# An mLSTM, dense and routed layer kernel on one core: one block's table scatters, one slot's rows and one slot's second layer put at other places of their queues

## What is computed

```
# 1. gated recurrent attention, 4 x 8 heads, 768 steps, head size 40
C = f * C + i * outer(v_t, k_t);  n = f * n + i * k_t
y_t = sigmoid(o_t) * (C @ q_t) / max(|n . q_t|, 1)
# 2. dense layer on x = y as 3072 tokens x 320
h = x @ w_in                        # 320 -> 2048
g = where(h >= 1, h, where(h <= -1, 0, (h + 1)**2 / 4))
x2 = g @ w_out                      # 2048 -> 320
# 3. routed layer: each token goes to the best of 8 experts
e = argmax(x2 @ w_gate);  p = softmax(x2 @ w_gate)[e]
out = p * (relu(x2 @ w1[e]) @ w2[e])   # 320 -> 1024 -> 320
```

## Time and profile before

| | |
|---|---|
| median of 3 runs | 816.65 us (814.5, 816.65, 816.67) |
| the profiled execution | 823.59 us, its span 821.4 us |
| PE busy in the span | 768.7 us (94%) |
| DVE, ACT, POOL busy | 595.2 (72%), 422.9 (51%), 318.5 us (39%) |
| PE clock, mean of the span | 0.988 of full |

### The profile page before, as it was taken

The page is one execution under the profiler, slowest core; times in us unless marked ns, Lnnn a source line. Parts: engine busy times, 40 slices in busy tenths (PEclk is TensorE's granted clock), DMA queues, the critical chain, the costliest instruction groups (busy, mean ns, idle before and its releaser), DMA issues. The chain is left out here.

```text
span 821.4 us, 17203 instructions
## 1 busy us (share of the span) xinstructions
PE 768.7 (94%) x5765; PEld 746.8 (91%) x5765; DVE 595.2 (72%) x1009; ACT 422.9 (51%) x649; POOL 318.5 (39%) x297
## 2 busy tenths in 40 slices
PE   2789999999999999999999999988979899999994
PEld 1788999999999999999999999988979899999994
DVE  4653768787878787878878788648677857676751
ACT  3022545454545454545454545663466766666761
POOL 3341543545343434454544444541434141313111
PEclk9999999999999999999999999998989999999998
DMA  6962222222222222222323210566647554338400
GB/s 198 308 174 75 75 93 76 90 75 90 74 90 74 90 74 93 81 95 85 94 87 92 83 40 1 174 160 171 236 145 228 205 198 158 121 94 266 148 7 5
DMA packets 41458, 97.05 MB, mean 118 GB/s; under 512 B 6936, under 2 KB 24482, under 8 KB 39755
## 3 DMA queue, kind: packets, MB, share of 16 engines
q1 hardware_dynamic: 37498, 87.46, 34.0%
q0 software_dynamic: 3920, 9.08, 3.6%
HBM read 105.63 MB, written 9.33 MB: 140 GB/s over the span
## 5 line engine op out<-in xcount | busy, mean ns | idle before, releaser
L552 POOL TENSOR_TENSOR g_t<-u_t,r_t 128x512 f32<-128x512 f32 x96 | 135.7, 1414 | 257.0 <-ACT u_t L702 256.9
L697 ACT ACTIVATE r_t<-bank,neg 128x512 f32<-128x512 f32 x96 | 66.0, 688 | 189.9 <-PE bank L1446 189.9
L1458 PE MATMUL bank<-wo_h,g_h 128*128 128x328 f32 x384 | 127.2, 331 | 0.0
L1033 DVE TENSOR_SCALAR u_t<-bank 128x512 f32<-128x512 f32 x96 | 66.1, 688 | 76.2 <-ACT r_t L697 49.2
L1458 PE MATMUL bank<-wo_h,g_l 128*128 128x328 f32 x384 | 120.2, 313 | 0.0
L1458 PE MATMUL bank<-wo_l,g_h 128*128 128x328 f32 x384 | 120.1, 313 | 0.0
L634 POOL DMA_INDIRECT out_x<-ob,idx_tok x31 | 37.4, 1208 | 153.8 <-ACT ob L772 149.5
L702 ACT ACTIVATE u_t<-u_t,half 128x512 f32<-128x512 f32 x96 | 69.5, 724 | 39.6 <-DVE u_t L1033 38.0
L969 DVE TENSOR_TENSOR_SCAN W<-W,cst 128x512 f32<-128x512 f32 x48 | 83.2, 1737 | 5.0 <-DMA W<-decays 5.0
L1579 PE MATMUL bank<-w_h,h_h 128*128 128x320 f32 x248 | 79.4, 320 | 7.4 <-DVE w_l L1097 6.3
L1446 PE MATMUL bank<-xT_h,wi_h 128*128 (+1 forms) x384 | 79.5, 289 | 1.6 <-issue 1.6
(11 more groups left out here) (234 smaller groups left out, 1949.9 us busy)
## 6 DMA issues: line engine op xcount, KB each, us to landing
raw<-in_w SPq DMA_DIRECT2D x10, 1280.0 KB
W<-decays SPq DMA_DIRECT2D x24, 512.0 KB, 5.0
raw2n<-in_w SPq DMA_DIRECT2D x9, 1280.0 KB
raw<-in_w SPq DMA_DIRECT2D x10, 1024.0 KB
raw1n<-in_w SPq DMA_DIRECT2D x9, 1024.0 KB
raw<-in_w SPq DMA_DIRECT2D x20, 256.0 KB
raw1n<-in_w SPq DMA_DIRECT2D x18, 256.0 KB
qG<-in_q SPq DMA_DIRECT2D x24, 180.0 KB
```

Source lines behind the costliest of these rows:

```text
L552: pool.tensor_tensor(g_t[p % 2][:, :], u_t[p % 2][:, :], r_t[p % 2][:, :], ALU.add).then_inc(sm["g_done"], 1)
L697: act.activation(r_t[p % 2][:, :], bank_h[p % 2][:, :], ACT.Relu, bias=neg1[:, 0:1]).then_inc(sm["r_done"], 1)
L1033: dve.tensor_scalar(u_t[p % 2][:, :], bank_h[p % 2][:, :], 1.0, -1.0, ALU.min, ALU.max).then_inc(sm["u_done"], 1)
L1458: mm = pe.matmul(bank_acc[tt][:, 0:DL], l[p % 4][:, c], r[:, f, :], start=f == 0 and a == 0, stop=f == NT1 - 1 and a == 2)
```

## The change

Three orders are changed; no instruction is added, removed or resized.

1. **Scatters of block 10.** `to_table(10)` stood behind `gated(11, 7)`, the last of POOL's eight sums of the last block. It stands behind `gated(11, 6)` now, ahead of that sum. In all other blocks it stays.
2. **Slot 3 and slot 4.** The second layer of slot 2 was divided into tiles 0 to 2, 3 to 5 and 6 to 7 around `turn_y(3)` and `first2(3)`, `turn_y(4)`. It is divided into 0 to 2, 3 to 4 and 5 to 7. On DVE `y_low(4)` goes ahead of `h_low(3, 3)`.
3. **Slot 6.** On ACT and on DVE the split of its rows (`y_high(6)`, `y_low(6)`) goes ahead of the split of its first weights (`w1_high(6, .)`, `w1_low(6, .)`).

```diff
@@ POOL, body
                     if not att and p in (4, 5):
                         gather(p - 4)
-                if prev:
+                    if not att and p == 6:
+                        to_table(t - 1)
+                if prev and att:
                     to_table(t - 1)
@@ ACT
             h_high(5, 3)
+            y_high(6)
             w1_high(6, 0)
             w1_high(6, 1)
             for s in range(5, NS):
...
-                if s + 1 < NS:
+                if 6 < s + 1 < NS:
                     y_high(s + 1)
@@ DVE
             w1_low(4, 0)
+            y_low(4)
             h_low(3, 3)
-            y_low(4)
             w1_low(4, 1)
...
             h_low(5, 3)
+            y_low(6)
             w1_low(6, 0)
             w1_low(6, 1)
             for s in range(5, NS):
-                if s + 1 < NS:
+                if 6 < s + 1 < NS:
                     y_low(s + 1)
@@ PE, tail
                 turn_y(3)
-                second2(2, range(3, 6))
+                second2(2, range(3, 5))
                 first2(3)
                 turn_y(4)
-                second2(2, range(6, NT2))
+                second2(2, range(5, NT2))
                 first2(4)
```

## The result

The changed kernel took 811.49 us (median of 13 runs, 809.33 to 816.3) beside 817.2 us for the kernel before (13 runs, 814.5 to 823.08). The ratio is 0.9929, with a 95% interval of 0.9908 to 0.995: faster by 0.7%, 5.7 us. Forecast were 8.4 us and 808.3 us. The time lies inside 804.5 to 812.5 us, to which the prediction gave some 8 in 10 and more, and 1.0 us above the narrower 806 to 810.5 us that stands with the forecast. On two other chips the ratio was 0.9921 and 0.9919. The recorded execution went from 821.4 us of span to 814.1, by 7.3 us.

What follows compares the result with a forecast made beforehand. PE, busy 94% of the span, bounds the kernel, so its waits and half-clock stretches count. Gains of 5.5 + 2.7 + 0.2 + 0.0 = 8.4 us take 816.65 to 808.3 us (806 to 810.5; wider 804.5 to 812.5).

Steps and rivals of the forecast that it cites:

- Where part 1 acts, and how: Block 10's scatters start at 537.99 and 539.30; `second2(0)` starts without waiting at 552.3, not 557.83: 5.5 us gained.
- The delay of `gated(11, 7)`: On POOL this sum starts at 540.4, not 539.77, and PE loses the 0.6 us; bounds 0 and 1.7 us.
- The landing: Block 10's scatters must land by 549.4; at 7.7 us they land at 547.0, 2.4 us to spare.
- The rival of a late landing: Block 10's scatters still take 12.34 us and land at 551.6; 810.5 us, or 813.2 with the clock lost; chance 0.11.
- the slower one: Landing set by SP's loads, POOL's issues delay PE 1.7 us, more half clock at slot 3; 819.3 us; chance 0.03.
- The clock behind `second2(0)`: Without the wait ahead of `second2(0)` the clock stays at 2.4 GHz there: 2.7 us gained.
- The size of the wait: The profiled 6.1 us wait of `second2(0)` and its half-clock stretch were taken as gains of 5.5 and 2.7 us.
- a clock lost at slot 6: The broken wait around `first2(6)` loses the clock, costing one more stretch of 2.9 us; 811.2 us; chance 0.10.
- The cost of recording: The profiled execution lies some 7 us above the median, taken as recording cost, the same for both kernels.
- Part 2: Slots 3 and 4: `first2(3)` waits 3.7 us without gain or loss; gain at `first2(4)` capped at 0.2 us.
- Part 3: Slot 6: the 2.4 us wait breaks into about 0.4, 1.9 and 0.8 us; gain 0.0, up to 0.6 us.
- the case that before loses its clock at this wait in other runs: Slot 6: some runs of before lost the clock there and the broken wait keeps it; 805.5 us; chance 0.06.

Runs made afterwards that it cites:

- split kernel: Changed kernel with the second scatter of block 10 issued behind `gated(11, 7)`, the first ahead of it; 804.98 us (ratio 0.9895) and 804.58 us (0.9900) on two chips.
- after, again: The changed kernel, unedited, run once more on a second chip; 807.22 us beside 813.38 us for the kernel before, ratio 0.9921.
- Part 2 alone: Kernel before with only the orders of slots 3 and 4 changed; 811.82 us beside 811.7 us, ratio 0.9996.
- part 3 alone: Kernel before with only the order of slot 6 changed; 811.02 us beside 811.7 us, ratio 0.9982.
- after, third: The changed kernel, unedited, run on a third chip; 805.56 us beside 812.41 us for the kernel before, ratio 0.9919.
- part 1 alone: Kernel before with only the scatters of block 10 moved; 807.58 us beside 811.7 us, ratio 0.9933.
- split without parts 2 and 3: Kernel before with one scatter of block 10 ahead of `gated(11, 7)`, one behind, slots 3, 4 and 6 unchanged; 807.15 us, ratio 0.9938.
- the load behind: Kernel before with SP's load of the first weights of slot 1 issued behind the store of block 11; 812.56 us beside 813.38 us, ratio 0.9981.

## Why the prediction was right, and where it was off

**Where part 1 acts, and how: right.** POOL's scatters at 538.23 and 539.54 (forecast 538.0 and 539.3), 0.82 us after `pair_ready` (535.77 + 1.64 = 537.41), as forecast; no idle time at the copy into `pair`; `second2(0)` at 552.32 (forecast 552.3), at the full clock, with 48 products in 7.2 us. The second scatter began inside `g_low(11, 6)`, took 1.08 us and ended 0.85 us behind it (540.62 and 539.77), which is what the prediction had taken over from the long issue.

**The delay of `gated(11, 7)`: 1.15 us, not 0.6.** From the first product of `first(11, 7)` it starts 539.77 - 534.97 = 4.80 us later in before and 540.65 - 534.68 = 5.97 us later in after, and `second2(0)` 17.65 in place of the 16.50 of the split kernel. My step counted the two issues and took `pair_ready` over unchanged. It comes 2.73 us after that first product in after and 2.20 in before, so it is later by 0.5 us, and the cause lies 5 us upstream. POOL and DVE, before:

```profile
531.17 1.30 POOL L552 TENSOR_TENSOR g_t<-u_t,r_t 128x512 f32<-128x512 f32 x1
532.62 0.97 POOL L581 DMA_INDIRECT xg<-x_scratch,idx_tok  x1 [0.15 <-issue]
...
535.85 1.29 POOL L552 TENSOR_TENSOR g_t<-u_t,r_t 128x512 f32<-128x512 f32 x1 [0.62 <-ACT u_t L702]
```

```profile
531.18 1.32 DVE L1072 TENSOR_SCALAR ssum<-ssum 128x2 f32<-128x2 f32 x1
...
532.62 1.79 DVE L1091 TENSOR_TENSOR w_l<-raw,w_h 128x1536 fp32r<-128x1536 f32 x1
```

The same in after:

```profile
530.88 1.33 POOL L552 TENSOR_TENSOR g_t<-u_t,r_t 128x512 f32<-128x512 f32 x1
532.36 2.44 POOL L581 DMA_INDIRECT xg<-x_scratch,idx_tok  x1 [0.15 <-issue]
```

```profile
530.88 0.17 DVE L1075 TENSOR_SCALAR ssum<-ssum 128x2 f32<-128x2 f32 x1
...
532.20 1.76 DVE L1094 TENSOR_TENSOR w_l<-raw,w_h 128x1536 fp32r<-128x1536 f32 x1 [0.96 <-ACT w_h L730]
```

In before DVE's tiny `ssum` step starts 0.01 us behind POOL's sum and is held until that ends (532.50 and 532.47). In after it starts with the sum, takes 0.17 us, and so `w1_low` comes 0.16 us ahead of the gather and not with it, and the gather's issue takes 2.44 us. POOL's next sum is late by that, and the conversion into `dsti` is held until it ends: 1.64 us, to 537.41, where the sum ends at 536.07 + 1.30 = 537.37. In before it is held as well, for 0.96 us to 537.17, where the sum ends at 537.14. So `pair_ready` was never a time of DVE's own. In all thirteen profiles it comes 0.02 to 0.04 us behind the end of `gated(11, 6)`, and what delays that sum delays the scatters. All six profiles with both scatters ahead of the sum have this long gather and the conversion of 1.64 us, all seven of the other kernels have a short gather and 0.95 or 0.96 us, on all chips. Why the two engines meet 0.01 us differently at a place that the change does not touch, the runs do not say. In the recorded execution it did not show in `second2(0)`, and that 552.3 was met to 0.02 us is luck: the dense layer happened to be 0.3 us sooner (534.68 for 534.97), and I had counted from the end of `turn_y(1)`, while `second2(0)` starts 0.25 us ahead of it (552.57).

**The landing.** By 548.70 at the latest, inside the limit of 549.4. In the five other profiles with this order the second scatter landed 3.6 to 4.1 us after its start, where the prediction had allowed 7.7. The landings issued from 500 us on in "after, again" answer to the earlier trace rows:

```profile
DMA to landing us min/median/max: 3.8/4.7/9.4
```

The 9.4 us are those of block 11, for which `second2(0)` does not wait. The rival of a late landing did not come true, nor did the slower one.

**The clock behind `second2(0)`: 2.4 us, 2.7 forecast** (9.54 against 7.17 us in the table).

**The size of the wait: the term that was mis-sized.** My sum took 6.12 us of wait and one long half-clock stretch from a single execution. Part 2 alone and part 3 alone, which have before's order here, had 3.81 and 4.73 us, and lost 1.6 and 1.4 us to the clock. Against those, part 1 gains 20.56 - 17.65 + 8.68 - 7.12 = 4.5 us and 21.47 - 17.65 + 8.51 - 7.12 = 5.2 us, and not 8.2. This explains most of the distance between 8.4 and the 5.7 to 6.9 us that the three chips gave. The median of 811.49 us also lies near the numbers of two rivals (811.2 for a clock lost at slot 6, 810.5 for a late landing); neither happened in the three profiles of the changed kernel, so that nearness says nothing for them.

**The cost of recording: wrong.** I took the 7 us between the recorded execution and the median as recording. In the eleven later profiles the recorded run was between 1.1 us below its kernel's median (804.47 us in "after, third", median 805.56) and 3.4 us above it, 0.5 us above on average. The first two profiles are longer by 7 us in the table's third column. Both executions were slow in the routed layer, for a reason that stays open, and that of before had the longest wait too.

**Part 2: right in size** (0.25 us by profile, 0.2 forecast). The wait ahead of `first2(3)` was 5.3 us and not 3.7. It was not mainly a wait for DVE's place in the list, as I had read it, but for signals that came late, in before already; elsewhere it is 0.4 us.

**Part 3: right in its mechanism, wrong for the kernel.** The pieces were 0.64 and 1.60 us (0.4, 1.9 and 0.8 forecast). ACT began the split of w2 when its load landed, as forecast:

```profile
638.36 1.27 ACT L738 ACTIVATE w_h<-raw 128x1280 fp32r<-128x1280 f32 x1 [1.11 <-DMA raw<-in_w]
```

It landed 7.24 us sooner than before, and `second2(5)` started 7.24 us sooner, while `second2(4)`, ahead of the wait, started 6.60 us sooner (629.71 for 636.31). So 0.64 us were gained in between, the "up to 0.6" of the forecast for a transfer that lands sooner. In part 3 alone that stretch took 14.99 us, as in before (15.01), and gave nothing. But I gave 0.06 to the case that before loses its clock at this wait in other runs, and it was a frequent one: 1.5 us with part 1, lost in three of five profiles that have this wait of 2.4 us (part 1 alone, split without parts 2 and 3, the load behind) and kept in two (before, part 2 alone). The sum that would have been right is 4.5 to 5.2 for part 1, 0.25 and up to 1.5: 4.8 to 7.0 us.

## What to carry to other kernels

A short transfer that gates the next piece of work belongs ahead of the bulk load on the same DMA engines, and of a group of them only as many as must land, since each issue delays what stands behind it on that queue. Before a wait read in one trace becomes a term of a sum, ask how it would vary: a wait for a DMA landing beside a load was 3.8, 4.7 and 6.1 us in three executions, while the stretch up to `second2(0)` repeated to 0.02 us once no late transfer stood in it. A wait that sometimes loses TensorE's clock is worth breaking up even where the trace at hand shows it kept.

## What the runs showed of the hardware

- Stretches at 1.2 GHz at a wait lasted 3.41 or 6.83 us. The waits were 2.4 to 6.1 us long, and their length alone does not tell which it is: waits of 2.81 us (before, ahead of `first2(3)`) and 4.49 us (the load behind) gave 6.83, one of 4.73 us (part 3 alone) gave 3.41. The same wait of 2.40 us, in the same place of the list, kept the clock twice and lost it three times.
- The issue of an indirect DMA took 2.43 to 2.45 us where it began some 0.15 us into a split of 128x1536 elements with two inputs in SBUF, whatever the DMA was (a scatter in before, a gather in after), and ended some 0.85 us behind the split. Where it began within 0.01 us of the split it took 0.96 or 0.97 us, and the split 1.79 or 1.80 in place of 1.75 or 1.76. For the splits this is the contention that the Trainium skill tells of (GPSIMD Engine Reference, Key points).
- It goes the other way too: steps of DVE on 128x2 elements that take 0.17 us alone took 0.96, 1.32 and 1.64 us beside a sum of POOL that had begun before them, and ended 0.02 to 0.04 us behind it. These steps have one tensor input; whether they ran in the two-port mode that the Trainium skill names there beside two inputs, no run shows.
- In the first two profiles PE's signal for the turned rows of slot 3 stands 4.3 and 5.5 us behind the record of the product while the DMA engines were full; in the eleven others it stands 0.01 or 0.02 us behind, with DMA engines as full.
